# Long matrix products without a reader in the waits of a chunked delta-rule attention, ahead of two MoE layers

## What is computed

```python
for t in range(S):
    kt, vt, bt = (k_n[:, :, t], v[:, :, t], beta[:, :, t, None])
    y[:, :, t] = np.einsum('bhd,bhde->bhe', q[:, :, t], state)
    v_old = np.einsum('bhde,bhd->bhe', state, kt)
    state = state + bt[:, :, :, None] * np.einsum('bhd,bhe->bhde', kt, vt - v_old)
```

## Time and profile before

| | |
|---|---|
| median of 3 runs | 2302.71 us (2301.67 to 2304.5) |
| profiled execution | 2305.67 us, of which its span 2303.9 us |
| mean granted clock of TensorE | 0.988 |
| PE busy | 2220.0 us (96%), 15456 products |
| DVE, ACT, POOL busy | 1014.6 us (44%), 742.1 us (32%), 687.8 us (30%) |
| 50 to 100 us | PE busy 35.69, granted clock 0.93 |
| 100 to 150 us | PE busy 44.43, granted clock 0.66 |

### The profile page before, as it was taken

The page is one execution under the profiler, slowest core; times in us unless marked ns, Lnnn a source line. Parts: engine busy times, 40 slices in busy tenths (PEclk is TensorE's granted clock), DMA queues, the critical chain, the costliest instruction groups (busy, mean ns, idle before and its releaser), DMA issues.

```text
span 2303.9 us, 40703 instructions
## 1 busy us (share of the span) xinstructions
PE 2220.0 (96%) x15456; PEld 1845.1 (80%) x15456; DVE 1014.6 (44%) x1641; ACT 742.1 (32%) x1286; POOL 687.8 (30%) x506
## 2 busy tenths in 40 slices
PE   3899998999999999999999999999999999999998
PEld 3788886888888888888888888888888877888887
DVE  8877742643232322322232323232323246767676
ACT  4666542311111111111111111111111126666665
POOL 2100001004432323233332323232323244444433
PEclk9889999999999999999999999999999999999999
DMA  6343333102111011111101111111110100000001
GB/s 160 100 105 98 87 88 118 55 28 55 39 31 29 27 46 32 27 32 27 45 28 32 27 32 27 45 29 30 30 29 27 46 23 14 14 14 14 0 14 69
DMA packets 85221, 102.35 MB, mean 44 GB/s; under 512 B 8384, under 2 KB 70144, under 8 KB 85120
## 3 DMA queue, kind: packets, MB, share of 16 engines
q1 hardware_dynamic: 85120, 100.91, 15.9%
HBM read 87.40 MB, written 8.75 MB: 42 GB/s over the span
## 4 chain that ended last, share of the span: by engine, by line
PE 75%; issue 12%; POOL 6%; DVE 5%; ACT 1%; SPq 1%; DMA 0%; POOLq 0%; DVEq 0%; ACTq 0%
PE p_h L605 5%; PE h L605 5%; PE p_h L606 5%; PE h L606 5%; PE h L607 5%; PE p_h L607 5%; POOL hlo L1116 5%; PE am_y L634 4%; PE am_y L635 4%; PE am_y L636 4%; PE chain_y L634 2%; PE chain_y L635 2%; PE chain_y L636 2%; PE o_y L634 2%; PE o_y L635 2%
## 5 line engine op out<-in xcount | busy, mean ns | idle before, releaser
L1095 POOL TENSOR_TENSOR acc<-acc,py 128x512 f32 (+1 forms) x252 | 325.2, 1321 | 744.4 <-DVE py L1439 744.4
L957 ACT ACTIVATE hhi<-h 128x512 fp32r<-128x512 f32 x182 | 109.0, 599 | 769.5 <-PE h L607 769.5
L1406 DVE SCALAR_TENSOR_TENSOR hlo<-h,hhi 128x512 fp32r<-128x512 f32 x182 | 125.9, 692 | 475.1 <-ACT hhi L957 475.0
L1406 DVE SCALAR_TENSOR_TENSOR hlo<-p_h,hhi 128x512 fp32r<-128x512 f32 x182 | 125.9, 692 | 406.7 <-ACT hhi L957 406.7
L1054 POOL TENSOR_TENSOR wlo<-stage,whi (+1 forms) x117 | 160.4, 1373 | 440.5 <-ACT whi L845 415.6
L605 PE MATMUL h<-xhi,whi 128*128 (+1 forms) x690 | 269.7, 391 | 2.9 <-DVE scr L1507 2.9
L605 PE MATMUL p_h<-xhi,whi 128*128 (+1 forms) x690 | 269.2, 390 | 0.1
L606 PE MATMUL h<-xlo,whi 128*128 (+1 forms) x690 | 269.2, 390 | 0.0
L607 PE MATMUL h<-xhi,wlo 128*128 (+1 forms) x690 | 269.1, 390 | 0.0
L607 PE MATMUL p_h<-xhi,wlo 128*128 (+1 forms) x690 | 268.5, 389 | 0.0
L606 PE MATMUL p_h<-xlo,whi 128*128 (+1 forms) x690 | 268.5, 389 | 0.0
(11 more groups left out here) (242 smaller groups left out, 4078.1 us busy)
## 6 DMA issues: line engine op xcount, KB each, us to landing
stage<-wcat SPq DMA_DIRECT2D x40, 768.0 KB, 4.4
pb<-p_scratch SPq DMA_DIRECT2D x84, 256.0 KB, 4.6
kq<-kqt SPq DMA_DIRECT2D x48, 192.0 KB, 3.4
kn<-krow SPq DMA_DIRECT2D x6, 768.0 KB, 6.2
kT<-kta SPq DMA_DIRECT2D x24, 192.0 KB, 5.3
v<-vrow SPq DMA_DIRECT2D x24, 192.0 KB, 4.2
kb<-krow SPq DMA_DIRECT2D x24, 192.0 KB, 4.9
out<-acc SPq DMA_DIRECT2D x6, 768.0 KB, 3.8
```

The lines of the kernel that those rows point to most:

```text
L957: act.activation(hhi[:, j, :], hps[j % 2][:, 0:TILE], ACT.Relu).then_inc(s["hhi_done"], 1)
L1095: pool.tensor_tensor(y, y, py[:, d, :], ALU.add).then_inc(s["added"], 1)
L1406: dve.scalar_tensor_tensor(out=hlo[:, j, :], in0=hps[j % 2][:, 0:TILE], scalar=0.0, in1=hhi[:, j, :].bitcast(F32), op0=ALU.max, op1=ALU.su ...
```

## The change

A table says for seven of the first eight steps how many products of 512 columns PE issues at the place of `beside_residual` and at that of `beside_update`: 43 in all. They multiply 128 columns of whi0 by the first 512 of whi0 and write o_ps; each starts anew, and nobody reads the result.

```diff
+UNREAD = {(0, 0): (0, 4), (0, 1): (3, 4), (0, 2): (7, 2), (0, 3): (6, 0),
+          (1, 0): (3, 0), (1, 1): (3, 4), (1, 2): (7, 0)}
...
+        def unread(n):
+
+            for _ in range(n):
+                pe.matmul(o_ps[:, :], w1(whi, 0, 0, 0), whi0[:, 0:TILE], start=True, stop=True)
+
         def beside_residual(g, c):
 
+            if (g, c) in UNREAD:
+                unread(UNREAD[g, c][0])
             if g >= 2 and c == 0:
                 early_up(g - 2, 3)
...
         def beside_update(g, c):
 
+            if (g, c) in UNREAD:
+                unread(UNREAD[g, c][1])
             if g >= 2 and c == 0:
                 early_gate(g - 2)
```

## The result

| | us |
|---|---|
| change, median of 18 runs | 2299.43 (2294.11 to 2303.08) |
| before, median of 18 runs beside it | 2302.62 (2298.38 to 2309.59) |
| ratio | 0.9983, 95% interval 0.9975 to 0.9991 |
| profiled execution of the change | 2301.13, of which its span 2299.4 |
| mean granted clock in it | 0.995 (0.988 before) |

What follows compares the result with a forecast made beforehand. PE was taken to set the end almost throughout, with DVE waiting for it at half clock. Terms 1.7 + 3.9 + 3.2 + 2.8 = 11.6 us, less 1.0, gave 10.6: 2292.1 us from the median, range 2288.0 to 2298.0.

Steps and rivals of the forecast that it cites:

- (0,2): Group 0, step 2: two groups of small PE products that DVE waits for run at full clock, 1.7 us gained.
- (0,3): Group 0, step 3: five small-product groups on PE's path shrink at full clock, 3.9 us gained.
- (1,0): Group 1, step 0: PE's path shrinks by 3.6 us net, but DVE's own work limits the gain to 3.2 us.
- (1,1): Group 1, step 1: DVE is busy without a break and the clock is already full, 0 gained.
- (1,2): Group 1, step 2: two small-product groups give 1.65 us and the nine of early_up 1.15, together 2.8 us.
- SP's queue: Moves of y and loads, near 19 us per two steps, were feared to take back the lead but would fit in 20.6.
- The fall in the merges: After (0,3)'s last long product, one short half-clock spell among merges and small groups, costing 0 to 1.7 us, taken as 1.0.
- 1 (a clock that stays down): Clock falls in the merges and stays down into (1,0); about 6.5 us gained, 2296.2 us; chance 0.17.
- Rival 2: Only idle time lowers the clock, so only the terms 1.7 and 2.8 remain: 2298.2 us; chance 0.05.
- Rivals 3 and 4: 3: no change, small products hold the clock down, 2302.7, chance 0.06; 4: slower, products don't lift the clock, 2307.7, chance 0.05.

Runs made afterwards that it cites:

- e3: The change with its 43 products cut from 512 to 64 columns: 2303.25 us, ratio 1.0004 to the kernel before.
- e11: The change with SP's moves of y halved in groups 0 and 1 and 5 and 6 more products in two later waits: 2296.72 us, ratio 0.9974.
- e7: The kernel before, without added products, with all of SP's moves of y split in halves: 2308.95 us, ratio 1.0024.
- e8: The kernel before, unedited, run once for a third profile: 2301.01 us for that execution.
- e9: The change with SP's moves of y halved in groups 0 and 1 alone: 2299.39 us, ratio 0.9982 to the kernel before.
- e2: The change, unedited, run again for a second profile: 2299.20 us, ratio 0.9986 to the kernel before.
- e6: The change without the three products of (1,0): 2299.34 us, ratio 0.9984 to the kernel before.
- e5: The change with all of SP's moves of y split in halves: 2305.83 us, ratio 1.0004 to the kernel before.

## Why the prediction was wrong

**The mechanism was right in its main part.** Products of 512 columns in the waits keep the clock up, and the time comes from DVE's waits for PE. e3 shows that their length matters (64 columns: ratio 1.0004), not whether by the work or by the pause that it closes. e11 shows the sum: 79.4 to 68.2 us is 11.2, for 11.6 at a clock that never falls.

Term by term, against the profile shown of before:

- (0,2): 1.7 foretold, 1.60, 1.57 and 1.58 measured in the three profiles of the change.
- (0,3): 3.9 foretold, 3.8, 3.1 and 3.8 measured.
- (1,0): **3.2 foretold, 0.4, 2.6 and 1.4 measured.** Here the step failed that counted PE's path in products alone. PE had to be given its instructions too. With small groups at full clock it uses up a block of 256 in 3.6 to 3.9 us by the count in the traces (128 products, 29 ns apart), at half clock in 5.0 to 5.9 us. Faster PE, same fetch, as e7 shows too: the change made PE fast enough to run into it, 1.8 us on average off this term, some of it by a fall of the clock behind the stop. e11 without the stop has 10.46 us, the sum's number.
- (1,1): 0 foretold; it took 0.1 longer.
- (1,2): 2.8 foretold, 2.8, 2.8 and 2.8 measured.
- SP's queue, the one I feared, held the lead of PE back nowhere by itself. Its traffic may be what the blocks of instructions stood behind; that is not shown.

**The step that failed most is the first one: what was subtracted from what.** The prediction read one profile, found 41 us of half clock in it, wrote "so long products bring the level back, and small ones alone don't hold it", and took the whole sum off the median of 2302.71 us. e8 refutes the sentence: small products alone brought the level back at 112 us and held it for 24 us. The rows that the prediction itself shows spoke against it as well, with the rises at 96.6 and 127.3 us. Six profiles of before need 76.3 us on average for the way that took 79.4 in the one I used: 3.1 us of the 10.6 were not there to be won on average. Two thirds of that, 2.1 us, lie in (1,0)-(1,1): it takes 11.6 us on average over the six and 12.3 over the three profiles of the change, so of the 3.2 us foretold nothing was won there, while (0,2), (0,3) and (1,2) brought 1.6, 3.0 and 2.4. The hint was on the table: the profiled time lay 3 us above the median. I named it and then took the median as "what other runs will be measured by" without taking those 3 us off the gain.

**The rest.** The fall in the merges, for which I took off 1.0 us, came in e9, at the place foretold; in the change itself the falls came after the stop, and between R of (1,3) and R of (2,0), where before lost nothing in five profiles of six and the change lost 1.5 and 2.3 us in two of three. From R of (0,1) to L466 the six profiles of before take 319.8 us and the three of the change 314.8: 5.0 us, to the 3 to 4 of the timed runs. The difference fits the choice of executions: the six profiled ones of before have a mean of 2305.2 us, over 2 us above the median of all runs of before (2302.85), and the three of the change 2299.2, near theirs (2299.58). So even the six are a slow sample, and 3.1 us may be too little. With so few profiles, each up to 4 us from their mean, this split is good to 1 or 2 us.

Small slips of the prediction change none of this: the low end of its range is 2302.7 less 12.5 and 1.8, which is 2288.4 and not 2288.0, and the first four products, in (0,0), ran ahead of the records of the clock, 2.07 us for the four, so at half clock.

Of the rivals, 1 (a clock that stays down) describes e9, but not the main cause. Rival 2 (only idle time lowers the clock) is refuted by e9's fall with PE busy. Its 2298.2 us is the nearest of all the numbers to the 2299.43 measured, but by luck. Rivals 3 and 4 are out by the ratio. That the profile shown could be an unusual one, and that instructions could come late, were no rivals of mine, and should have been.

## What to carry to other kernels

A single profile is one draw. Where a gain rests on a state that can differ between executions of one program, such as the granted clock, take it off that profile's own time, and if that time lies above the median, count the distance against the gain. When a change makes an engine run through small instructions faster, look for idle time put down to issue, and count the instructions between two such places: here they were 256 apart, the engine's instructions came in blocks of that size, and a block could be late while the DMA engines were busy. Filling waits on TensorE with long products was worth 3 to 4 us of 2302.6 for 43 products, and 7 with more waits filled and the transfers spread.

## What the runs showed of the hardware

- The granted clock of one program differs from execution to execution: half clock from 100.0 to 127.3 us in one, 101.7 to 112.0 in another, 100.5 to 121.0 in a third, over the same instructions. It can rise and fall among small products with PE busy for 8 us and more before (e8: busy from 103.9, rise at 112.0; e9: busy from 102.2, fall at 111.2).
- Late blocks of instructions stop TensorE for 0.4 to 1.8 us at fixed counts of its instructions, 256 apart, in kernels with and without the added products (e2, e7), and the place in the program moves by as many products as are taken out ahead of it (24 to 27 in e6).
- Transfers run in the order in which SP issues them: ten more behind a reload that waits made the pause behind the attention 6.3 us longer in e5 and e7.
